# A block's MLP issued over four slots and a bit instead of ten

## The chip, the cores and the metric

The kernel runs on one core of a Trainium2 chip. The metric is the device time of one execution in microseconds. The engines of a core run their own instruction streams side by side and wait for each other on semaphores: TensorE (PE) does matmuls, VectorE (DVE), ScalarE (ACT) and GpSimd (POOL) work on tiles, and SyncE (SP) issues the transfers.

## What is computed

Attention with 4 batches, 8 heads, 576 positions and head size 64, in which each query keeps its 32 highest scores only, and behind it an MLP over 2304 tokens of width 512 with 2048 hidden values:

```python
scores = scale * np.matmul(q, k.transpose(0, 1, 3, 2))
kth = np.partition(scores, -top_k, axis=-1)[..., -top_k:-top_k + 1]
scores = np.where(scores >= kth, scores, -1000000000.0)
attn = np.exp(scores - max) ; attn = attn / (sum + 1e-09)
x = (attn @ v) of all heads side by side       # 2304 x 512
h = x @ w_in                                   # 2304 x 2048
g = h * np.tanh(log1p(exp(h)))                 # mish
y = g @ w_out                                  # 2304 x 512
```

## The kernel before

**Tiling.** The 2304 tokens are 18 blocks of 128 (`BLOCKS`). A block has four duos (`PPB`), each the 128 queries of two heads, so there are 72 duos (`DUOS`). The loops run over slots. In slot s each engine does one stage of several duos at once: PE computes `scores(s+2)` and transposes the finished weights of duo s-3 (`transposes`); ACT copies scores from PSUM (`copy_x(s+2)`), makes the penalty of duo s-1 (`penalties`), its exponentials (`exps`) and copies the transposed weights of duo s-3 (`copy_pT`); DVE does the whole `topk(s)` and one reciprocal (`inverse(s-2)`); POOL turns duo s-1's 32nd score into a limit (`negate`), subtracts (`exponents(s-1)`), adds 1e-9 to the sum (`guard`), multiplies the weights of duo s-2 by the reciprocal (`normalise`), and makes low parts of q and k (`split_q`, `split_k`). `values` of two duos (weights times v) stand together in every even slot. Blocks 4 and 13 are mixed: their 128 queries come from two batches, and their scores use all 128 rows of the array.

**The MLP of a block.** When its four duos are done, `copy_xT` brings x into SBUF; `up(m, j)`, j = 0 to 3, are 16 fp32 matmuls each (32 passes in a profile), written into two PSUM buffers in turn; `copy_up` moves a group to `g_raw`; `mish` works on each half; `split_g(m, h)` makes a rounded high part and a low part of a half (a cast and a subtraction on POOL); `down(m, j)` are 12 matmuls of 512 columns each; `copy_y` and `store` bring the result out. `ps_y` and `y_sb` are single.

**What sets the order.** Every engine's order is written out by hand, slot by slot, and each executes in that order. Before, `UP_SLOT` = 6 puts up(0, 0) in slot 6 and one further up into each slot; `MISH_SLOT` = 10 puts both halves of mish at the end of slot 10, 14, ...; the halves are split on POOL in the two slots after it; `DOWN_SLOT` = 12 puts one down group into each slot from 12 on. So a block's MLP stretches over slots 4m+6 to 4m+15. At slot 74 the slots end, and behind them stand down(15, 3), the last three ups, and the downs of blocks 16 and 17.

**Loads of new keys.** When a batch is done, `split_k` makes the high part of new keys on ACT and the low part on POOL at the end of slots 14, 15, 30 to 33, 50 and 51 (two in each of 14, 15, 50 and 51, one in the others).

Of the kernel before, what the change touches and what calls it, by code (L numbers as in the profile page):

```python
# [40 lines left out]

UP_SLOT, MISH_SLOT, DOWN_SLOT = 6, 10, 12
WCHUNKS = 8
# [59 lines left out]

STAGED = PPB


# [8 lines left out]
def program(nc, k_in, q_in, v, w_in, w_out, y_out):  # L115
    with ExitStack() as ctx:
# [77 lines left out]
        ghi_ready = sem("ghi_ready")  # L194
        glo_ready = sem("glo_ready")
        down_ready = sem("down_ready")
        y_copied = sem("y_copied")
# [23 lines left out]
        def _(sp):  # L221
# [51 lines left out]
            for k in range(KC):  # L273
                sp.dma_start(win[:, k, :], w_in[P * k:P * k + P, :]).then_inc(win_loaded, 16)
            for s in range(DUOS + DOWN_SLOT):
                if STAGED < s + 3 < DUOS:
                    load_q(s + 3)
                for c in w_chunks_at(s - 1):
                    if c + 2 < WCHUNKS:
                        load_w(c + 2)  # L280
                for g in splits_at(s - 1):
                    if PPB <= g and g + RAWS < PAIRS:
                        load_k(g + RAWS)
                for pr in range(PPB):
                    for i in range(1, len(V_USES[pr])):
                        if values_slot(V_USES[pr][i - 1][3]) == s:
                            load_v(pr, i)
                m, j = divmod(s - DOWN_SLOT, GROUPS)
                if j == GROUPS - 1 and 0 <= m < BLOCKS:
                    store(m)  # L290
# [3 lines left out]
        def _(pe):  # L294
# [82 lines left out]
            def down(m, j):  # L377
                if m == 0 and j == 0:
                    pe.wait_ge(wlo_ready, WCHUNKS)
                if j == 0 and m >= 1:  # L380
                    pe.wait_ge(y_copied, m)
                if j % 2 == 0:
                    pe.wait_ge(glo_ready, 2 * m + j // 2 + 1)
                for f in range(FPG * j, FPG * j + FPG):
                    for g, w in ((g_hi, w_hi), (g_hi, w_lo), (g_lo, w_hi)):
                        mm = pe.matmul(ps_y[:, :], g[:, f, :], w[:, f, :],  # L386
                                       start=(f == 0 and g is g_hi and w is w_hi), stop=(f == FT - 1 and g is g_lo),
                                       skip_group_check=True)
                mm.then_inc(down_ready, 1)

            pe.wait_ge(ident_ready, 1)
            for s in range(-2, DUOS + LAG_PT):
                if s >= LAG_PT:
                    transposes(s - LAG_PT)
                m, j = divmod(s - DOWN_SLOT, GROUPS)
                if m >= 0:
                    down(m, j)
                for d in (s - LAG_PT - 1, s - LAG_PT):
                    if d >= 0 and values_slot(d) == s:
                        values(d)  # L400
                if s + 2 < DUOS:
                    scores(s + 2)
                m, j = divmod(s - UP_SLOT, GROUPS)
                if m >= 0:
                    up(m, j)
            down(BLOCKS - 3, 3)
            for j in range(1, GROUPS):
                up(BLOCKS - 1, j)
            for j in range(GROUPS):
                down(BLOCKS - 2, j)  # L410
            for j in range(GROUPS):
                down(BLOCKS - 1, j)

        @block.scalar
        def _(act):
# [67 lines left out]
            def copy_up(m, j):  # L483
                n = GROUPS * m + j
                act.wait_ge(up_ready, n + 1)
                if n == 0:
                    act.wait_ge(wlo_ready, WCHUNKS)
                if j % 2 == 0 and m >= 1:

                    act.wait_ge(glo_ready, 2 * (m - 1) + j // 2 + 1)  # L490
                act.activation(g_raw[:, FPG * j:FPG * j + FPG, :], ps_u[:, n % 2, :, :],
                               ACT.Copy).then_inc(up_copied, 1)

            def mish(m):
                for h in range(2):
                    act.wait_ge(up_copied, GROUPS * m + 2 * h + 2)
                    g = g_raw[:, FT // 2 * h:FT // 2 * h + FT // 2, :]
                    act.activation(g, g, ACT.Mish).then_inc(mish_ready, 1)

# [8 lines left out]
            split_k(1)  # L508
            for s in range(-2, DUOS + LAG_PT):
                if s >= LAG_PT:  # L510
# [5 lines left out]
                m, j = divmod(s - UP_SLOT - 1, GROUPS)  # L516
                if m >= 0:
                    copy_up(m, j)
                if s >= LAG_PT and (s - LAG_PT) % PPB == PPB - 1:
                    copy_xT((s - LAG_PT) // PPB)  # L520
                if 0 <= s + 2 < DUOS:
                    copy_x(s + 2)
                m, j = divmod(s - DOWN_SLOT, GROUPS)
                if m >= 0 and j == GROUPS - 1:
                    copy_y(m)
                if 0 <= s - LAG_EXP < DUOS:
# [4 lines left out]
                for c in w_chunks_at(s):  # L531
                    split_w(c)
                m, j = divmod(s - MISH_SLOT, GROUPS)
                if m >= 0 and j == 0:
                    mish(m)
            copy_up(BLOCKS - 1, 0)
            copy_y(BLOCKS - 3)
            for j in range(1, GROUPS):
                copy_up(BLOCKS - 1, j)
            mish(BLOCKS - 1)  # L540
            copy_y(BLOCKS - 2)
            copy_y(BLOCKS - 1)

        @block.vector
        def _(dve):
# [4 lines left out]
            def topk(s):  # L550
# [8 lines left out]
                for r in range(TOPK // EIGHT - 1):  # L559
                    for t in range(2):  # L560
                        if r == 0:
                            dve.wait_ge(top8_ready, 2 * s + t + 1)
                        else:
# [4 lines left out]
                                          imm_value=NEG).then_inc(found, 1)  # L568
                    if r == 0 and s >= LAG_NORM:
                        inverse(s - LAG_NORM)  # L570
# [10 lines left out]
            for s in range(DUOS - LAG_NORM, DUOS):  # L581
                inverse(s)

        @block.gpsimd
        def _(pool):
# [57 lines left out]
            split_k(1)  # L643
            for s in range(-2, DUOS + LAG_NORM):
                if 0 <= s - LAG_EXP < DUOS:
                    negate(s - LAG_EXP)
                m, j = divmod(s - MISH_SLOT - 1, GROUPS)
                if m >= 0 and j < 2:
                    split_g(m, j)
                for c in w_chunks_at(s - 1):  # L650
                    split_w(c)
                if 0 <= s - LAG_NORM:
                    normalise(s - LAG_NORM)
                if 0 <= s - LAG_EXP < DUOS:
                    exponents(s - LAG_EXP)
                if s + 3 < DUOS:
                    split_q(s + 3)
                if 0 <= s - LAG_EXP < DUOS:
                    guard(s - LAG_EXP)
                if s > -2:  # L660
                    for g in splits_at(s):
                        split_k(g)
            for m in range(BLOCKS - 2, BLOCKS):
                for h in range(2):
                    split_g(m, h)

# [38 lines left out]
```

## Time and profile before

| | us |
|---|---|
| median of 3 runs | 783.95 (783.53 to 784.21) |
| profiled execution, device time | 782.78 |
| its span in the trace | 781.0 |
| PE busy | 717.6 (92%) |
| PE weight loads busy | 641.7 (82%) |
| DVE busy | 700.3 (90%) |
| ACT busy | 546.1 (70%) |
| POOL busy | 546.3 (70%) |

The span runs from the first to the last instruction of the trace, and the device time has some 1.8 us around it. The shares are averages over the whole span: DVE works only while there are duos, PE also behind them. So the slots (where both are busy) and the end (where only PE is) are to be read apart. The mean granted clock of PE over the profile is 0.986 of full speed.

### The profile page before, as it was taken

To read this page: it belongs to the slowest core of one execution; us is meant where nothing else is said; L and a number is where in the kernel's file an instruction comes from. 1 tells how busy PE (TensorE), PEld (TensorE's weight loads), DVE (VectorE), ACT (ScalarE), POOL (GpSimd) and SP (SyncE) were. 2 spreads that over 40 slices of the span, in tenths; PEclk is the share of its full clock that TensorE was granted. 3 is DMA by queue.
4 is the path that set the end of the run, shared out by engine and by line. 5 is a ranking of instruction groups with operands and counts; after the bars stand their busy time and mean duration, and the time that the engine had idled before them with its cause. 6 is when DMAs were issued, how large, how long until landed. Compare 5 with 4: busy or idle time off the path is not lost.

```text
span 781.0 us, 16741 instructions
## 1 busy us (share of the span) xinstructions
PE 717.6 (92%) x6280; PEld 641.7 (82%) x6280; DVE 700.3 (90%) x1513; ACT 546.1 (70%) x994; POOL 546.3 (70%) x677
## 2 busy tenths in 40 slices
PE   2257759999999999999999999999999999999998
PEld 2246758988888888888888888988888888889896
DVE  6999999998999999999999999998999999996000
ACT  4677666776868687878686878686868686867420
POOL 3977568697767676887676768687767776767333
PEclk9987999999999999999999999999999999999999
DMA  9521000031121000211100000020122000000000
GB/s 346 185 62 34 8 8 12 15 115 40 59 85 45 8 22 10 52 38 54 42 23 8 23 8 21 16 77 23 56 75 90 8 22 8 21 2 14 2 14 28
DMA packets 22689, 34.64 MB, mean 44 GB/s; under 512 B 2384, under 2 KB 11600, under 8 KB 22096
## 3 DMA queue, kind: packets, MB, share of 16 engines
q1 hardware_dynamic: 22608, 33.56, 13.4%
q8 instruction: 50, 0.82, 0.4%
q14 instruction: 31, 0.25, 0.1%
HBM read 28.84 MB, written 4.72 MB: 43 GB/s over the span
## 4 chain that ended last, share of the span: by engine, by line
PE 55%; DVE 32%; POOL 4%; ACT 4%; issue 4%; DMA 1%; SPq 0%; ACTq 0%; POOLq 0%
PE ps_u L373 22%; PE ps_y L386 16%; DVE left L565 15%; DVE top L573 12%; PE ps_s L314 5%; PE ps_s L332 5%; PE ps_o L357 5%; DVE top L558 5%; POOL p_sb L624 1%; PE ps_o L350 1%; ACT p_sb L464 1%; POOL g_lo L610 1%; ACT pT L473 1%; POOL p_sb L635 1%; POOL k_lo L588 1%
## 5 line engine op out<-in xcount | busy, mean ns | idle before, releaser
L573 DVE MAX8 top<-left 128x8 f32<-128x576 f32 x432 | 305.2, 751 | 0.0
L373 PE MATMUL ps_u<-xT,win 128*128 128x128 f32 x2304 | 275.6, 278 | 2.6 <-ACT xT L481 2.6
L373 PEld LDWEIGHTS ps_u<-xT,win 128*128 128x128 f32 x2304 | 263.9, 192 | 13.0 <-issue 9.2
L565 DVE MATCH_REPLACE8 left<-top,left 128x576 f32<-128x576 f32 x288 | 212.5, 748 | 0.0
L624 POOL TENSOR_TENSOR p_sb<-x_sb,p_sb 128x576 f32<-128x576 f32 x144 | 200.8, 1416 | 0.0
L464 ACT ACTIVATE p_sb<-p_sb,neg_max 128x576 f32<-128x576 f32 x144 | 111.3, 775 | 62.0 <-POOL p_sb L624 61.5
L635 POOL TENSOR_SCALAR p_sb<-p_sb,recip 128x576 f32<-128x576 f32 x144 | 106.2, 748 | 51.0 <-DVE recip L548 51.0
L386 PE MATMUL ps_y<-w_hi,g_hi 128*128 128x512 f32 x288 | 119.0, 413 | 0.7 <-ACT y_sb L504 0.7
L445 ACT ACTIVATE x_sb<-ps_s 128x576 f32<-128x576 f32 x144 | 85.6, 648 | 48.0 <-PE ps_s L314 47.8
L386 PE MATMUL ps_y<-w_hi,g_lo 128*128 128x512 f32 x288 | 113.0, 392 | 0.0
L386 PE MATMUL ps_y<-w_lo,g_hi 128*128 128x512 f32 x288 | 112.3, 390 | 0.0
L456 ACT ACTIVATE p_sb<-x_sb,limit 128x576 f32<-128x576 f32 x144 | 103.5, 770 | 8.2 <-POOL limit L615 8.2
L565 DVE MATCH_REPLACE8 left<-top,x_sb 128x576 f32<-128x576 f32 x144 | 106.3, 749 | 0.0
L558 DVE MAX8 top<-x_sb 128x8 f32<-128x576 f32 x144 | 101.4, 748 | 3.0 <-ACT x_sb L445 3.0
L473 ACT ACTIVATE pT<-ps_s 128x512 f32<-128x512 f32 (+1 forms) x144 | 84.6, 638 | 23.3 <-PE ps_s L332 23.3
L332 PE MATMUL ps_s<-ident,p_sb 128*128 128x128 f32 x648 | 85.7, 279 | 8.8 <-POOL p_sb L635 7.6
L610 POOL TENSOR_TENSOR g_lo<-g_raw,g_hi 128x1024 fp32r<-128x1024 f32 x36 | 86.0, 2389 | 3.1
L357 PEld LDWEIGHTS ps_o<-pT,v_sb 128*64 128x64 f32 x1280 | 72.0, 141 | 18.1 <-issue 13.7
L357 PE MATMUL ps_o<-pT,v_sb 128*64 128x128 f32 x1280 | 80.9, 282 | 6.1 <-ACT pT L473 6.1
L332 PEld LDWEIGHTS ps_s<-ident,p_sb 128*128 128x128 f32 x648 | 75.2, 144 | 10.4 <-ACT x_sb L445 5.9
L314 PE MATMUL ps_s<-k_hi,q_hi 64*128 64x288 f32 (+1 forms) x288 | 43.1, 362 | 42.1 <-ACT pT L473 21.4
L314 PEld LDWEIGHTS ps_s<-k_hi,q_hi 64*128 64x128 f32 (+1 forms) x288 | 25.5, 199 | 60.4 <-issue 43.6
(41 smaller groups left out, 730.1 us busy)
## 6 DMA issues: line engine op xcount, KB each, us to landing
v_sb<-v_in SPq DMA_DIRECT2D x32, 320.0 KB, 3.6
g_raw<-w_out SPq DMA_DIRECT2D x8, 512.0 KB, 3.8
win<-w_in SPq DMA_DIRECT2D x4, 1024.0 KB, 11.8
y_out<-y_sb SPq DMA_DIRECT2D x16, 256.0 KB, 2.0
k_raw<-k_in SPq DMA_DIRECT2D x14, 288.0 KB, 2.9
q_raw<-q_in SPq DMA_DIRECT2D x60, 64.0 KB, 1.8
q_raw<-q_in SPq DMA_DIRECT2D x8, 128.0 KB, 2.1
p_sb<-k_in SPq DMA_DIRECT2D x2, 288.0 KB, 5.2
```

The costliest lines, as they stand in the source:

```text
L314: mm = pe.matmul(ps_s[:, t, h, 0:HALF], q[r, s % QS, c:c + P], k[r, g % PPB, HALF * h:HALF * h + HALF], start=first, stop=final, skip_grou ...
L332: mm = pe.transpose(flat[:, P * k:P * k + P], p[:, P * k:P * k + P], ident[:, :])
L357: mm = pe.matmul(ps_o[D * h:D * h + D, j, :], v_sb[:, j, k, D * h:D * h + D], pT[:, s % 2, SPLIT_AT * h + k, :], start=(k == 0), stop=(k = ...
L373: mm = pe.matmul(ps_u[:, n % 2, i, :], win[:, k, P * f:P * f + P], xT[:, k, :], start=(k == 0), stop=(k == KC - 1), skip_group_check=True)
L386: mm = pe.matmul(ps_y[:, :], g[:, f, :], w[:, f, :], start=(f == 0 and g is g_hi and w is w_hi), stop=(f == FT - 1 and g is g_lo), skip_gr ...
L456: act.activation(p_sb[:, s % PS_, t, :], x_sb[:, s % XS, t, :], ACT.Relu, bias=limit[:, s % TS, t:t + 1], scale=-BLOW_UP).then_inc(penalty ...
L464: act.activation(p, p, ACT.Exp, bias=neg_max[:, s % TS, t:t + 1], scale=SCALE, accum_out=denom[:, s % TS, t:t + 1]).then_inc(exp_ready, 1)
L558: dve.max(best[:, t, 0:EIGHT], x[t]).then_inc(top8_ready, 1)
L565: dve.match_replace(out=left[:, t, :], in_to_replace=best[:, t, EIGHT * r:EIGHT * r + EIGHT], in_values=x[t] if r == 0 else left[:, t, :], ...
L573: dve.max(best[:, t, EIGHT * r + EIGHT:EIGHT * r + 2 * EIGHT], left[:, t, :]).then_inc(found, 1)
L624: pool.tensor_tensor(p, x_sb[:, s % XS, t, :], p, ALU.subtract).then_inc(arg_ready, 1)
L635: pool.tensor_scalar(p, p, recip[:, s % TS, t:t + 1], 1.0, ALU.mult, ALU.mult).then_inc(p_ready, 1)
```

## The change

The MLP of block m now takes slots 4m+6 to 4m+9 and the start of slot 4m+10. `mlp_at(s)` gives the block and its slot r, 0 to 3. PE does up 0 at the end of the first slot, up 1 and up 2 in the second, up 3 in the third, down 0, 1 and 2 in the fourth, and down 3 at the start of the next block's first slot. ACT copies groups 0 and 1 and does the first half's mish at the end of the second slot, copies groups 2 and 3 and does the other half's between `copy_x` and `exps` in the third. POOL splits one half in the third and one in the fourth slot. The second half of the last block is split on DVE, whose duos are done. On POOL, `guard` moves from the end of a slot to the start of the next one, and `normalise` stands behind `exponents` except in the third slot; on DVE `inverse` moves one pair of passes back. `copy_y`, `store` and the first waits on `w_out` are moved with them.

```diff
-UP_SLOT, MISH_SLOT, DOWN_SLOT = 6, 10, 12
+MLP_SLOT, MLP_SLOTS = 6, 4
+def mlp_at(s):
+
+    m, r = divmod(s - MLP_SLOT, MLP_SLOTS)
+    return (m if 0 <= m < BLOCKS else None), r
+SLOTS = MLP_SLOT + MLP_SLOTS * BLOCKS + 1
...
-            for s in range(-2, DUOS + LAG_PT):
-                if s >= LAG_PT:
+            for s in range(-2, SLOTS):
+                m, r = mlp_at(s)
+                before, last = mlp_at(s - 1)
+                if LAG_PT <= s < DUOS + LAG_PT:
                     transposes(s - LAG_PT)
-                m, j = divmod(s - DOWN_SLOT, GROUPS)
-                if m >= 0:
-                    down(m, j)
-                for d in (s - LAG_PT - 1, s - LAG_PT):
-                    if d >= 0 and values_slot(d) == s:
+                if before is not None and last == 3:
+                    down(before, 3)
+                if m is not None and r == 1:
+                    up(m, 1)
+                if m is not None and r == 2:
+                    up(m, 3)
+                if m is not None and r == 3:
+                    down(m, 0)
+                two = [d for d in (s - LAG_PT - 1, s - LAG_PT) if 0 <= d < DUOS and values_slot(d) == s]
+                if r != 2:
+                    for d in two:
                         values(d)
                 if s + 2 < DUOS:
                     scores(s + 2)
-                m, j = divmod(s - UP_SLOT, GROUPS)
-                if m >= 0:
-                    up(m, j)
-            down(BLOCKS - 3, 3)
-            for j in range(1, GROUPS):
-                up(BLOCKS - 1, j)
-            for j in range(GROUPS):
-                down(BLOCKS - 2, j)
-            for j in range(GROUPS):
-                down(BLOCKS - 1, j)
+                if r == 2:
+                    for d in two:
+                        values(d)
+                if m is not None and r == 0:
+                    up(m, 0)
+                if m is not None and r == 1:
+                    up(m, 2)
+                if m is not None and r == 3:
+                    down(m, 1)
+                    down(m, 2)
...
+                if before is not None and last == 3:
+                    copy_y(before)
+                if m is not None and r == 0:
+                    copy_xT(m)
+                if m is not None and r == 1:
+                    copy_up(m, 0)
+                    copy_up(m, 1)
+                    if s >= DUOS + LAG_PT:
+                        mish(m, 0)
+                if m is not None and r == 2:
+                    copy_up(m, 2)
+                    copy_up(m, 3)
                 if 0 <= s + 2 < DUOS:
                     copy_x(s + 2)
-                m, j = divmod(s - DOWN_SLOT, GROUPS)
-                if m >= 0 and j == GROUPS - 1:
-                    copy_y(m)
+                if m is not None and r == 2:
+                    mish(m, 1)
                 if 0 <= s - LAG_EXP < DUOS:
                     exps(s - LAG_EXP)
...
-                m, j = divmod(s - MISH_SLOT, GROUPS)
-                if m >= 0 and j == 0:
-                    mish(m)
...
+                if m is not None and r == 1 and s < DUOS + LAG_PT:
+                    mish(m, 0)
...
-                    if r == 0 and s >= LAG_NORM:
+                    if r == 1 and s >= LAG_NORM:
                         inverse(s - LAG_NORM)
...
+            g, f = BLOCKS - 1, slice(FT // 2, FT)
+            dve.wait_ge(mish_ready, 2 * g + 2)
+            dve.wait_ge(down_ready, GROUPS * g)
+            dve.tensor_copy(g_hi[:, f, :], g_raw[:, f, :]).then_inc(ghi_last, 1)
...
-                m, j = divmod(s - MISH_SLOT - 1, GROUPS)
-                if m >= 0 and j < 2:
-                    split_g(m, j)
+                if 0 <= s - LAG_NORM < DUOS:
+                    guard(s - LAG_NORM)
+                if m is not None and r == 2:
+                    split_g(m, 0)
+                if m is not None and r == 3 and m < BLOCKS - 1:
+                    split_g(m, 1)
                 for c in w_chunks_at(s - 1):
                     split_w(c)
-                if 0 <= s - LAG_NORM:
+                if r == 2 and 0 <= s - LAG_NORM < DUOS:
                     normalise(s - LAG_NORM)
                 if 0 <= s - LAG_EXP < DUOS:
                     exponents(s - LAG_EXP)
+                if r != 2 and 0 <= s - LAG_NORM < DUOS:
+                    normalise(s - LAG_NORM)
                 if s + 3 < DUOS:
                     split_q(s + 3)
-                if 0 <= s - LAG_EXP < DUOS:
-                    guard(s - LAG_EXP)
```

ACT, before: the slot in which both halves of mish stand, and the one behind it (`p_sb,denom` are the exponentials, `pT` the transposed weights, L491 copies an up group, L445 scores, L504 y).

```order
164 L491 ACTIVATE g_raw<-ps_u 128x512
165 L445 ACTIVATE x_sb<-ps_s 128x576 x2
166 L464 ACTIVATE p_sb,denom<-p_sb,neg_max 128x576 x2
...
182 L498 ACT_TABLE_LOAD
183 L498 ACTIVATE g_raw<-g_raw 128x1024 x2
184 L473 ACTIVATE pT<-ps_s 128x512
185 L473 ACTIVATE pT<-ps_s 128x640
186 L456 ACTIVATE p_sb<-x_sb,limit 128x576 x2
187 L434 ACTIVATE q_hi<-q_raw 128x128
188 L491 ACTIVATE g_raw<-ps_u 128x512
```

ACT, after: the end of a block's second slot and the whole third one (L523 is mish, L517 copies up groups, L470 scores, L489 the exponentials, L498 the transposed weights).

```order
190 L523 ACT_TABLE_LOAD
191 L523 ACTIVATE g_raw<-g_raw 128x1024
192 L498 ACTIVATE pT<-ps_s 128x512
193 L498 ACTIVATE pT<-ps_s 128x640
194 L481 ACTIVATE p_sb<-x_sb,limit 128x576 x2
195 L459 ACTIVATE q_hi<-q_raw 128x128
196 L517 ACTIVATE g_raw<-ps_u 128x512 x2
197 L470 ACTIVATE x_sb<-ps_s 128x576 x2
198 L523 ACTIVATE g_raw<-g_raw 128x1024
199 L489 ACT_TABLE_LOAD
200 L489 ACTIVATE p_sb,denom<-p_sb,neg_max 128x576 x2
```

One half of mish and the table load for the exponentials have moved between the copy of the scores and the exponentials of the third slot.

POOL, before: one of the two slots with a split of g (L608 and L610), then the start of the next (L635 is `normalise`, L624 `exponents`, L594 `split_q`, L628 `guard`, L615 and L617 `negate`).

```order
147 L615 TENSOR_SCALAR limit<-top 128x2
148 L617 TENSOR_SCALAR neg_max<-top 128x2
149 L608 CAST g_hi<-g_raw 128x1024
150 L610 TENSOR_TENSOR g_lo<-g_raw,g_hi 128x1024
151 L635 TENSOR_SCALAR p_sb<-p_sb,recip 128x576 x2
152 L624 TENSOR_TENSOR p_sb<-x_sb,p_sb 128x576 x2
153 L594 TENSOR_TENSOR q_lo<-q_raw,q_hi 128x128
154 L628 TENSOR_SCALAR denom<-denom 128x2
```

POOL, after: the fourth slot of a block (L648 and L650 are `negate`, L661 `guard`, L641 and L643 `split_g`, L657 `exponents`, L668 `normalise`, L627 `split_q`).

```order
156 L648 TENSOR_SCALAR limit<-top 128x2
157 L650 TENSOR_SCALAR neg_max<-top 128x2
158 L661 TENSOR_SCALAR denom<-denom 128x2
159 L641 CAST g_hi<-g_raw 128x1024
160 L643 TENSOR_TENSOR g_lo<-g_raw,g_hi 128x1024
161 L657 TENSOR_TENSOR p_sb<-x_sb,p_sb 128x576 x2
162 L668 TENSOR_SCALAR p_sb<-p_sb,recip 128x576 x2
163 L627 TENSOR_TENSOR q_lo<-q_raw,q_hi 128x128
```

`guard` (of the duo before) now stands ahead of the split, and `normalise` behind `exponents`.

DVE, after: its last instructions. Before, it ended with the two reciprocals.

```order
575 L598 MAX top<-left 128x8 x2
576 L573 RECIPROCAL recip<-denom 128x2 x2
577 L612 CAST g_hi<-g_raw 128x1024
578 L614 TENSOR_TENSOR g_lo<-g_raw,g_hi 128x1024
579 L127 UNCONDITIONAL_BRANCH
```

The split of the last half block has come behind them.

## Rows read from the trace of the kernel before

**Rows 1.** The page's chain that ended last; then DVE's longest wait (total, times, longest).

```profile
PE 55%; DVE 32%; POOL 4%; ACT 4%; issue 4%; DMA 1%; SPq 0%; ACTq 0%; POOLq 0%
...
DVE recip L548 <- POOL denom L628: 19.2, 7, 9.3
```

**Rows 2.** Timeline, PE, slots 67 and 68: start us, duration us, engine, line, operation, tiles.

```profile
667.98 1.15 PE L332 MATMUL ps_s<-ident,p_sb 128*128 128x128 f32 x9
...
671.83 0.53 PE L314 MATMUL ps_s<-k_hi,q_hi 64*128 64x288 f32 x4
...
672.82 3.84 PE L373 MATMUL ps_u<-xT,win 128*128 128x128 f32 x32
676.50 1.15 PE L332 MATMUL ps_s<-ident,p_sb 128*128 128x128 f32 x9
...
683.67 3.84 PE L373 MATMUL ps_u<-xT,win 128*128 128x128 f32 x32
687.34 1.15 PE L332 MATMUL ps_s<-ident,p_sb 128*128 128x128 f32 x9
```

**Rows 3.** Timeline, DVE: the first pass of topk in slots 9 and 10.

```profile
95.24 1.41 DVE L558 MAX8 top<-x_sb 128x8 f32<-128x576 f32 x2
104.94 1.41 DVE L558 MAX8 top<-x_sb 128x8 f32<-128x576 f32 x2
```

**Rows 4.** Timeline, PE, slots 11 and 12: idle time before an instruction in brackets.

```profile
117.62 0.70 PE L314 MATMUL ps_s<-k_hi,q_hi 64*128 64x288 f32 x4 [4.76 <-ACT pT L473]
...
123.83 1.15 PE L332 MATMUL ps_s<-ident,p_sb 128*128 128x128 f32 x9
```

**Rows 5.** The end: PE enters slot 70; the last copy of y.

```profile
695.86 1.15 PE L332 MATMUL ps_s<-ident,p_sb 128*128 128x128 f32 x9
...
777.97 0.60 ACT L504 ACTIVATE y_sb<-ps_y 128x512 f32<-128x512 f32 x1 [11.26 <-PE ps_y L386]
```

**Rows 6.** The chain in order of time: one down group.

```profile
124.98 2.76 PE ps_y L386 x12
```

**Rows 7.** Timeline, PE, slot 51: scores of a mixed block, and the up behind them.

```profile
513.94 0.77 PE L314 MATMUL ps_s<-k_hi,q_hi 128*128 128x288 f32 x4 [0.96 <-ACT pT L473]
...
515.65 3.73 PE L373 MATMUL ps_u<-xT,win 128*128 128x128 f32 x32
```

**Rows 8.** Timeline, slot 30: scores, their copies on ACT, the exponentials.

```profile
308.87 0.53 PE L314 MATMUL ps_s<-k_hi,q_hi 64*128 64x288 f32 x4
...
309.96 1.19 ACT L445 ACTIVATE x_sb<-ps_s 128x576 f32<-128x576 f32 x2 [0.38 <-PE ps_s L314]
...
311.04 0.78 ACT L464 ACTIVATE p_sb<-p_sb,neg_max 128x576 f32<-128x576 f32 x1
```

**Rows 9.** Timeline, ACT, slots 10 and 11: both halves of mish, the table load, exponentials.

```profile
114.40 2.00 ACT L498 ACTIVATE g_raw<-g_raw 128x1024 f32<-128x1024 f32 x2
...
121.92 1.28 ACT L464 ACT_TABLE_LOAD   x1 [1.12 <-POOL p_sb L624]
123.21 0.78 ACT L464 ACTIVATE p_sb<-p_sb,neg_max 128x576 f32<-128x576 f32 x1
```

**Rows 10.** Timeline, POOL, slot 11: split of g, normalise, exponents, split of q, guard.

```profile
115.52 1.04 POOL L608 CAST g_hi<-g_raw 128x1024 fp32r<-128x1024 f32 x1 [0.18 <-ACT g_raw L498]
...
119.00 1.47 POOL L635 TENSOR_SCALAR p_sb<-p_sb,recip 128x576 f32<-128x576 f32 x2
120.44 2.77 POOL L624 TENSOR_TENSOR p_sb<-x_sb,p_sb 128x576 f32<-128x576 f32 x2
123.17 0.46 POOL L594 TENSOR_TENSOR q_lo<-q_raw,q_hi 128x128 fp32r<-128x128 f32 x1
124.93 0.22 POOL L628 TENSOR_SCALAR denom<-denom 128x2 f32<-128x2 f32 x1 [1.30 <-ACT p_sb L464]
```

**Rows 11.** Timeline, slot 30: the split of new keys on ACT and POOL.

```profile
312.55 0.68 ACT L424 ACTIVATE k_hi<-k_raw 128x576 fp32r<-128x576 f32 x1
...
313.31 1.41 POOL L588 TENSOR_TENSOR k_lo<-k_raw,k_hi 128x576 fp32r<-128x576 f32 x1 [0.34 <-ACT k_hi L424]
```

More of the change, by code:

```diff
@@ L195, in program @@
         glo_ready = sem("glo_ready")
+        ghi_last = sem("ghi_last")
+        glo_last = sem("glo_last")
         down_ready = sem("down_ready")
@@ L274, in _ @@
                 sp.dma_start(win[:, k, :], w_in[P * k:P * k + P, :]).then_inc(win_loaded, 16)
-            for s in range(DUOS + DOWN_SLOT):
+            for s in range(SLOTS + 1):
                 if STAGED < s + 3 < DUOS:
@@ L287, in _ @@
                             load_v(pr, i)
-                m, j = divmod(s - DOWN_SLOT, GROUPS)
-                if j == GROUPS - 1 and 0 <= m < BLOCKS:
+                m, r = mlp_at(s - 1)
+                if m is not None and r == 3:
                     store(m)
@@ L381, in down @@
                     pe.wait_ge(y_copied, m)
-                if j % 2 == 0:
+                if j == 2 and m == BLOCKS - 1:
+                    pe.wait_ge(glo_last, 1)
+                elif j % 2 == 0:
                     pe.wait_ge(glo_ready, 2 * m + j // 2 + 1)
@@ L402, in _ @@
                     scores(s + 2)
-                m, j = divmod(s - UP_SLOT, GROUPS)
-                if m >= 0:
-                    up(m, j)
-            down(BLOCKS - 3, 3)
-            for j in range(1, GROUPS):
-                up(BLOCKS - 1, j)
-            for j in range(GROUPS):
-                down(BLOCKS - 2, j)
-            for j in range(GROUPS):
-                down(BLOCKS - 1, j)
+                if r == 2:
[5 more added lines that the diff above has]
+                    up(m, 2)
+                if m is not None and r == 3:
+                    down(m, 1)
+                    down(m, 2)
         @block.scalar
@@ L485, in copy_up @@
                 act.wait_ge(up_ready, n + 1)
-                if n == 0:
-                    act.wait_ge(wlo_ready, WCHUNKS)
+                if m == 0 and j % 2 == 0:
+                    act.wait_ge(wlo_ready, WCHUNKS - 1 + j // 2)
                 if j % 2 == 0 and m >= 1:
@@ L492, in copy_up, with mish @@
                                ACT.Copy).then_inc(up_copied, 1)
[L494 to L498, printed above, removed]
+            def mish(m, h):
+                act.wait_ge(up_copied, GROUPS * m + 2 * h + 2)
+                g = g_raw[:, FT // 2 * h:FT // 2 * h + FT // 2, :]
+                act.activation(g, g, ACT.Mish).then_inc(mish_ready, 1)
             def copy_y(m):
@@ L508, in _ @@
             split_k(1)
-            for s in range(-2, DUOS + LAG_PT):
-                if s >= LAG_PT:
+            for s in range(-2, SLOTS):
+                m, r = mlp_at(s)
+                before, last = mlp_at(s - 1)
+                if LAG_PT <= s < DUOS + LAG_PT:
                     copy_pT(s - LAG_PT)
@@ L515, in _ @@
                     split_q(s + 3)
[L516 to L520, printed above, removed]
+                if before is not None and last == 3:
[10 more added lines that the diff above has]
+                    copy_up(m, 3)
                 if 0 <= s + 2 < DUOS:
                     copy_x(s + 2)
-                m, j = divmod(s - DOWN_SLOT, GROUPS)
-                if m >= 0 and j == GROUPS - 1:
-                    copy_y(m)
+                if m is not None and r == 2:
+                    mish(m, 1)
                 if 0 <= s - LAG_EXP < DUOS:
@@ L532, in _ @@
                     split_w(c)
-                m, j = divmod(s - MISH_SLOT, GROUPS)
-                if m >= 0 and j == 0:
-                    mish(m)
[L536 to L542, printed above, removed]
+                if m is not None and r == 1 and s < DUOS + LAG_PT:
+                    mish(m, 0)
         @block.vector
@@ L582, in _ @@
                 inverse(s)
+            g, f = BLOCKS - 1, slice(FT // 2, FT)
+            dve.wait_ge(mish_ready, 2 * g + 2)
+            dve.wait_ge(down_ready, GROUPS * g)
+            dve.tensor_copy(g_hi[:, f, :], g_raw[:, f, :]).then_inc(ghi_last, 1)
+            dve.wait_ge(ghi_last, 1)
+            dve.tensor_tensor(g_lo[:, f, :], g_raw[:, f, :], g_hi[:, f, :].bitcast(F32),
+                              ALU.subtract).then_inc(glo_last, 1)
         @block.gpsimd
@@ L643, in _ @@
             split_k(1)
-            for s in range(-2, DUOS + LAG_NORM):
+            for s in range(-2, SLOTS):
+                m, r = mlp_at(s)
                 if 0 <= s - LAG_EXP < DUOS:
                     negate(s - LAG_EXP)
-                m, j = divmod(s - MISH_SLOT - 1, GROUPS)
-                if m >= 0 and j < 2:
-                    split_g(m, j)
+                if 0 <= s - LAG_NORM < DUOS:
[4 more added lines that the diff above has]
+                    split_g(m, 1)
                 for c in w_chunks_at(s - 1):
                     split_w(c)
-                if 0 <= s - LAG_NORM:
+                if r == 2 and 0 <= s - LAG_NORM < DUOS:
                     normalise(s - LAG_NORM)
@@ L662, in _ @@
                         split_k(g)
-            for m in range(BLOCKS - 2, BLOCKS):
-                for h in range(2):
-                    split_g(m, h)
 def kernel(q, k, v, moe_w_in, moe_w_out):
```

## The prediction

> **What bounds the kernel now.** I read the chain that ended last first [rows 1]: 55% PE and 32% DVE. Two engines share the bound, so the next thing to look at is their step. DVE starts a new duo every 9.70 us (104.94 - 95.24) [rows 3] and needs no pause between passes. PE, in a slot pair near the end, takes 687.34 - 667.98 = 19.36 us for two slots [rows 2], or 9.68 a slot. Both are full. DVE's wait for the reciprocal's input is 19.2 us in 7 waits, the longest (9.3) behind its last duo, so about 10 us lie among the duos [rows 1]. Then the end: PE enters slot 70 at 695.86, and y is copied for the last time at 777.97 [rows 5], which is 82.1 us of PE work with no topk beside most of it. The start is different: PE does no down group before slot 12, entered at 123.83, and waited 4.76 us in slot 11 [rows 4].
>
> So PE is the resource. The change takes no PE work away. It can gain only by filling PE's idle time before slot 12 and by avoiding later waits. It loses wherever its new order makes PE wait.
>
> **PE's pieces** from the same rows. A down group is 2.76 [rows 6]. Transposes are 671.83 - 667.98 - 2.76 = 1.09, scores 672.82 - 671.83 = 0.99, an up group 676.50 - 672.82 = 3.68, and values with scores 683.67 - 676.50 - 1.09 - 2.76 = 3.32, so values are 2.33 [rows 2].
>
> The slots of a block are then, in the new order: first 1.09 + 2.76 + 3.32 + 3.68 = 10.85; second 1.09 + 3.68 + 0.99 + 3.68 = 9.44; third 1.09 + 3.68 + 0.99 + 2.33 = 8.09; fourth 1.09 + 0.99 + 3 x 2.76 = 10.36. Sum 38.74, against 38.72 now and 38.80 of DVE. Per block nothing is gained or lost by itself. Check on before: slots 12 to 69 are 29 pairs, 561.4; eight scores of mixed blocks take 515.65 - 513.94 = 1.71 instead of 0.99 [rows 7], 5.8 more; PE's span there is 695.86 - 123.83 = 572.0, so some 4.8 us in 58 slots are waits. That is small: before, PE hardly waits in the slots.
>
> **The start.** In the new order PE enters slot 10 when POOL has normalised duo 7 in slot 9. From the start of slot 8 on DVE (95.24 - 9.70 = 85.54): the reciprocal stands behind 4 of 7 pairs of passes, 9.70 x 4/7 = 5.54, with itself 5.75; normalise 1.44; exponents 2.73, that is 9.9; the second exponential, with the way to guard, some 1.0; then guard 0.3, split of g 119.00 - 115.52 = 3.48, exponents 2.73, normalise 1.47 and 0.1 to the release [rows 10]. Sum 19.0, so slot 10 starts at 104.6; I take 104.8. With 3 down groups done by then, PE has work from there on.
>
> **The waits that the order brings.** This is the term that I am least sure of, so it is worked out step by step, from PE's entry into a block's third slot (0) to its entry into the next first slot. PE itself needs 8.09 + 10.36 = 18.45. The other way is through ACT and POOL:
> - up 3 and transposes, 4.77; scores start; the copy on ACT starts 309.96 - 308.87 = 1.09 later, 5.86; 311.04 - 309.96 = 1.08 for both copies, 6.94 [rows 8];
> - the half of mish that now stands there, 2.00 / 2 = 1.00, then the table load 123.21 - 121.92 = 1.29, 9.23 [rows 9];
> - from the first exponential to guard 124.93 - 123.21 = 1.72, 10.95 [rows 9, 10];
> - guard 0.3, which now stands ahead of the split and so holds POOL's whole fourth slot; split 3.48; exponents 2.73; normalise 1.47; release 0.1: 19.03 [rows 10].
>
> PE's transposes wait for that normalise. So PE loses 19.03 - 18.45 = 0.58 us per block. The same sum for the fourth slot's scores, which need the copied transposes (10.7 + 1.2 against 8.09 + 3.85), comes out even, and down 2, needing the second split at 14.7 against 15.7, doesn't wait. The 15 blocks from slot 10 to slot 70 pay it, less the two in which the longer mixed scores cover it: 13 x 0.58 = 7.5. Its bounds: below, nothing, since a sum of eleven durations can be off by 0.5 and some work may overlap more than in the rows; above, 1.2 per block if each hand-over costs a little more.
>
> **New keys.** Before, splits of keys fell on slots with a split of g. Now slots 14, 15, 30, 31, 50 and 51 have none. Only slot 32, a third one, is hit: POOL finishes its split of q at 9.6, waits for ACT's copy of the keys, which comes behind the exponentials (10.8 + 0.6), then works 1.41 [rows 11], to 12.9; negate and guard 0.9, and 3.48 + 2.73 + 1.57 give 21.6, against 18.45: 3.15, of which 0.58 is counted, so 2.6. The bounds are 0 and 4.
>
> **The end.** From slot 70 on PE has 8 up groups before and after, and 9 down groups (1, 3, 1, 4) instead of 14 (5 in slots 70 to 74, and 9): 5 x 2.76 = 13.8 less. The wait for the copy of y between the last two blocks, 0.7, goes as well. 82.1 - 14.5 = 67.6. New waits there: down 0 of the last block needs mish and split of the first half (copy 0.6, load 1.3, mish 1.0, split 3.5, together 6.4 behind up 1), while up 2 and up 3 cover 7.4; the other half needs 0.6 + 1.0 and two passes on DVE, some 2.4 by its 9.70 / 14 = 0.69 per 576 columns, covered by down 0 and 1 (5.5). Nothing is late there; without cover it would be 1 to 2 us. Slots 72 to 74 have no scores or exponents beside them, and POOL's sum is shorter than PE's. The stores keep their place behind copy_y.
>
> **Other edits at nothing.** The reciprocal, 2.8 us later, delays normalise; DVE itself is helped, since guard may come 2.8 us later before it waits. In a first or second slot normalise then ends some 7.4 us after DVE's start, more than 2 us before PE wants it. The number of table loads goes from 34 to 36, the same two a block; the last slots' are under PE's work. Transfers don't come earlier or later by more than a slot, and none is in the chain but 1%.
>
> **A rule against the change.** The rows show a switch of tables as 1.28 us, and the exponential begins 1.29 after the load began [rows 9]. The Trainium skill, ScalarE: Activation LUTs, section "What ACT_TABLE_LOAD costs", gives a load of about 1283 ns and a drain of about 1380 ns besides. The trace agrees on the first and shows no second part. It matters since the load now lies in the path that I summed.
>
> **Sum.** 104.8 + 15 x 38.72 (580.8) + mixed 5.8 + 7.5 + 2.6 = 701.5 at slot 70; + 67.6 = 769.1 at the last copy of y, against 777.97. The span ended 781.0 - 777.97 = 3.0 later: 772.1. The device time of the profiled execution is 1.8 above its span: 773.9. The median of the runs is 1.2 above that execution (783.95 - 782.78): **775.1**.
>
> **Rivals.**
> - *PE runs through* (27%). The chain above is shorter than PE's own 18.45, and nothing of 7.5 and 2.6 is paid: 765.0, and up to 770.5 with half of it. For it: the difference is only 0.58 in 19. Against it: before, behind slot 50 with mish and key splits together, PE already waited 0.96 us for ACT's copy of the transposes [rows 7].
> - *The chain as summed* (53%): 770.5 to 779.
> - *The chain is longer* (13% for 779 to 785.5, of which 4% lie within 0.2% of before; 7% beyond). The same guard-to-normalise chain in the third and fourth slot, with a price per block P instead of 0.58: the time is 765.0 + 2.6 + 13 P, and it passes 783.95 at P = 1.26, that is 0.7 us more in the chain than summed. It could come from ACT: in a second slot its copies, exponentials, load and mish end 4.77 + 1.09 + 1.08 + 1.72 + 1.29 + 1.00 = 10.95 after PE's entry, 1.5 behind PE's entry into the third [rows 8, 9, 10]. My estimate is that it catches up with some 0.7 us to spare; if it does not, all that I started from PE's scores starts later. An engine drain at each load, as long as the load itself, would be such a thing: 1.3 us in the chain, 14 times, and 775.1 + 18.2 = 793.3. No row shows one [rows 9], so I give it 1% of the 7. The Trainium skill, in the section named above, states such a drain.
>
> Slower beyond 0.2% is then 7%, same 4% and faster 89%. A measurement of this kernel can tell about 0.2%, 1.6 us, from no change. The range that holds 8 in 10: from 766 to 781; below it some 5%, above it 14%.
>
> **What would show it.** Right: PE enters the transposes of slot 10 near 105 and shows 12 down passes ahead of it; PE's transposes in each first slot show an idle time of about 0.6 released by POOL's normalise; DVE's last pass still ends near 716, since PE, and not DVE, sets the step; the time from slot 70 to the last copy of y is 67 to 69. The whole gain is then in the end, 14.5, less some 6 that slot 70 comes later than before. Wrong: PE has no idle time in the slots and slot 70 starts before 694 (first rival); or the waits at a block's first slot are over 1.2 and slot 70 starts after 708; or PE waits in the last block, between up 3 and down 0, which would mean that its cover is not there.

## The result and the profile after

| | before | after |
|---|---|---|
| median of 5 runs, us | 783.75 (783.03 to 784.21) | 779.51 (779.38 to 779.93) |
| profiled execution, device time | 782.78 | 779.93 |
| its span | 781.0 | 777.9 |
| PE enters slot 10 | 99.88 | 105.58 |
| PE enters slot 70 | 695.86 | 706.35 |
| last copy of y begins | 777.97 | 774.93 |

The ratio is 0.9948, with a 95% interval from 0.9933 to 0.9962. The change makes the kernel 4.2 us faster. The forecast was 8.9 us, so the sign and the range held, and the size was off by more than a factor of two.

The chain that ended last, on the page of the changed kernel, answers to [rows 1]:

```profile
PE 40%; POOL 34%; DVE 10%; ACT 10%; issue 5%; DMA 0%; ACTq 0%; SPq 0%; POOLq 0%
PE ps_u L386 16%; POOL p_sb L657 11%; POOL g_lo L643 10%; PE ps_y L401 9%; POOL p_sb L668 6%; DVE left L590 5%; PE ps_s L327 5%; PE ps_o L370 5%; PE ps_s L345 4%; POOL g_hi L641 4%; DVE top L598 4%; ACT p_sb L489 3%; ACT L523 2%; ACT g_raw L523 2%; DVE top L583 2%
```

POOL had 4% of the chain before and has 34% now. Its lines are the subtraction (L657), the split of g (L641, L643) and the normalising (L668): the work of a block's fourth slot. The waits of PE between slot 10 and slot 70 (for whom: total, times, longest) show the same:

```profile
PE ps_s L327 <- ACT pT L498: 6.7, 13, 1.5
PE ps_s L345 <- POOL p_sb L668: 5.6, 13, 1.3
PE ps_y L401 <- POOL g_lo L643: 0.8, 1, 0.8
```

PE waits 13.1 us there, against 4.8 between slots 12 and 70 before. One ordinary block, slots 46 to 50, in PE's timeline (start us, duration us, engine, line, operation, tiles, idle time before it):

```profile
466.65 1.18 PE L345 MATMUL ps_s<-ident,p_sb 128*128 128x128 f32 x9 [0.34 <-POOL p_sb L668]
477.49 1.15 PE L345 MATMUL ps_s<-ident,p_sb 128*128 128x128 f32 x9
486.81 1.15 PE L345 MATMUL ps_s<-ident,p_sb 128*128 128x128 f32 x9
494.78 1.20 PE L345 MATMUL ps_s<-ident,p_sb 128*128 128x128 f32 x9
498.94 0.53 PE L327 MATMUL ps_s<-k_hi,q_hi 64*128 64x288 f32 x4 [0.22 <-ACT pT L498]
506.03 1.17 PE L345 MATMUL ps_s<-ident,p_sb 128*128 128x128 f32 x9 [0.36 <-POOL p_sb L668]
```

The block takes 506.03 - 466.65 = 39.38 us. It would be 38.72 by [rows 2]. The first, second and third slot take 10.84, 9.32 and 7.97, none longer than in the sum; the fourth takes 11.25, and both idle times stand in or behind it. What ACT and POOL do in these microseconds:

```profile
493.63 1.06 ACT L523 ACTIVATE g_raw<-g_raw 128x1024 f32<-128x1024 f32 x1
494.80 1.28 ACT L489 ACT_TABLE_LOAD   x1
496.10 0.78 ACT L489 ACTIVATE p_sb<-p_sb,neg_max 128x576 f32<-128x576 f32 x1
...
497.63 1.17 ACT L498 ACTIVATE pT<-ps_s 128x512 f32<-128x512 f32 x2
```

```profile
497.81 0.22 POOL L661 TENSOR_SCALAR denom<-denom 128x2 f32<-128x2 f32 x1 [0.67 <-ACT p_sb L489]
498.09 1.04 POOL L641 CAST g_hi<-g_raw 128x1024 fp32r<-128x1024 f32 x1
499.21 2.42 POOL L643 TENSOR_TENSOR g_lo<-g_raw,g_hi 128x1024 fp32r<-128x1024 f32 x1
501.57 2.84 POOL L657 TENSOR_TENSOR p_sb<-x_sb,p_sb 128x576 f32<-128x576 f32 x2
504.38 1.50 POOL L668 TENSOR_SCALAR p_sb<-p_sb,recip 128x576 f32<-128x576 f32 x2
```

Mish, load, exponentials, guard (L661, after an idle time of 0.67), split, subtraction, normalise: 504.38 + 1.50 = 505.88, and PE's transposes begin at 506.03. It is the chain of the prediction, piece for piece: 506.03 - 486.81 = 19.22 us from PE's third slot on, 19.03 in the sum.

Two theories of the lost gain went to the chip. **A**: this chain over ACT and POOL, with normalise at its end, holds PE once a block. **B**: PE's and DVE's own steps set the pace, and the idle times would turn up elsewhere if they were removed; for the moved guard and reciprocal, B says that they are what makes four slots possible.

### The profile page after: what moved, and what is told of

Same layout as the page of the kernel before. It is cut to its first block, busy times and chain, and to the rows that moved or that the text cites. A ratio compares the mean times of both kernels' runs of the same rounds, so it can differ in the third digit from the quotient of the medians.

```text
span 777.9 us, 16744 instructions
## 1 busy us (share of the span) xinstructions
PE 715.6 (92%) x6280; PEld 642.4 (83%) x6280; DVE 703.2 (90%) x1515; ACT 552.8 (71%) x996; POOL 546.7 (70%) x675
## 3 DMA queue, kind: packets, MB, share of 16 engines
q1 hardware_dynamic: 22608, 33.56, 13.5%
## 4 chain that ended last, share of the span: by engine, by line
PE 40%; POOL 34%; DVE 10%; ACT 10%; issue 5%; DMA 0%; ACTq 0%; SPq 0%; POOLq 0%
PE ps_u L386 16%; POOL p_sb L657 11%; POOL g_lo L643 10%; PE ps_y L401 9%; POOL p_sb L668 6%; DVE left L590 5%; PE ps_s L327 5%; PE ps_o L370 5%; PE ps_s L345 4%; POOL g_hi L641 4%; DVE top L598 4%; ACT p_sb L489 3%; ACT L523 2%; ACT g_raw L523 2%; DVE top L583 2%
## 5 line engine op out<-in xcount | busy, mean ns | idle before, releaser
L386 PE MATMUL ps_u<-xT,win 128*128 128x128 f32 x2304 | 271.4, 276 | 1.4 <-ACT xT L506 1.4
L657 POOL TENSOR_TENSOR p_sb<-x_sb,p_sb 128x576 f32<-128x576 f32 x144 | 202.3, 1428 | 66.6 <-ACT p_sb L481 66.6
L489 ACT ACTIVATE p_sb<-p_sb,neg_max 128x576 f32<-128x576 f32 x144 | 110.8, 774 | 46.9 <-POOL p_sb L657 46.7
L498 ACT ACTIVATE pT<-ps_s 128x512 f32<-128x512 f32 (+1 forms) x144 | 85.4, 642 | 57.1 <-PE ps_s L345 57.1
L401 PE MATMUL ps_y<-w_hi,g_hi 128*128 128x512 f32 x288 | 117.2, 407 | 1.6 <-POOL g_lo L643 1.6
L668 POOL TENSOR_SCALAR p_sb<-p_sb,recip 128x576 f32<-128x576 f32 x144 | 106.9, 756 | 3.6 <-DVE recip L573 3.6
L470 ACT ACTIVATE x_sb<-ps_s 128x576 f32<-128x576 f32 x144 | 85.6, 647 | 26.4 <-PE ps_s L327 26.3
L643 POOL TENSOR_TENSOR g_lo<-g_raw,g_hi 128x1024 fp32r<-128x1024 f32 x35 | 83.8, 2393 | 3.0
L327 PE MATMUL ps_s<-k_hi,q_hi 64*128 64x288 f32 (+1 forms) x288 | 43.0, 359 | 34.6 <-ACT pT L498 14.5
L641 POOL CAST g_hi<-g_raw 128x1024 fp32r<-128x1024 f32 x35 | 36.4, 1039 | 47.2 <-ACT g_raw L523 45.8
```

Source lines behind the costliest of these rows:

```text
L386: mm = pe.matmul(ps_u[:, n % 2, i, :], win[:, k, P * f:P * f + P], xT[:, k, :], start=(k == 0), stop=(k == KC - 1), skip_group_check=True)
L401: mm = pe.matmul(ps_y[:, :], g[:, f, :], w[:, f, :], start=(f == 0 and g is g_hi and w is w_hi), stop=(f == FT - 1 and g is g_lo), skip_gr ...
L489: act.activation(p, p, ACT.Exp, bias=neg_max[:, s % TS, t:t + 1], scale=SCALE, accum_out=denom[:, s % TS, t:t + 1]).then_inc(exp_ready, 1)
L643: pool.tensor_tensor(g_lo[:, f, :], g_raw[:, f, :], g_hi[:, f, :].bitcast(F32), ALU.subtract).then_inc(glo_ready, 1)
L657: pool.tensor_tensor(p, x_sb[:, s % XS, t, :], p, ALU.subtract).then_inc(arg_ready, 1)
L668: pool.tensor_scalar(p, p, recip[:, s % TS, t:t + 1], 1.0, ALU.mult, ALU.mult).then_inc(p_ready, 1)
```

## Experiments

All are edits of the changed kernel. Each time is a median; block is PE's time from the first slot of an ordinary block to the next.

| run | us | block, us |
|---|---|---|
| changed kernel | 779.51 | 39.38 |
| x1_norm_first | 771.41 | 38.85 |
| x2_keys_later | 777.07 | 39.38 |
| x3_old_guard | 768.77 | 38.86 |
| x4_no_tables | 767.47 | 38.55 |
| x5_cast_twice | 798.67 | 40.48 |
| x8_guard_only | 783.63 | 39.85 |
| x7_guard_keys | 768.02 | 38.86 |
| x9_early_load | 766.03 | 38.83 |

**Normalise ahead of the subtraction in the fourth slot.**

```diff
-                if r == 2 and 0 <= s - LAG_NORM < DUOS:
+                if r >= 2 and 0 <= s - LAG_NORM < DUOS:
                     normalise(s - LAG_NORM)
...
-                if r != 2 and 0 <= s - LAG_NORM < DUOS:
+                if r < 2 and 0 <= s - LAG_NORM < DUOS:
                     normalise(s - LAG_NORM)
```

> Of the changed kernel, one edit: in a block's fourth slot POOL normalises before it subtracts (as in the third). Theory A, the chain over ACT and POOL holds PE back once per block: the normalise that PE's next transposes wait for ends 2.8 us earlier, the wait of 0.36 us at each block's first slot goes (and the 1.30 at slot 34), the 0.22 at the fourth slot's scores stays; a block goes from 39.38 to about 38.9 us, slot 70 starts some 7 us earlier, near 699, and the time is about 773. Theory B, the slot times are set by PE and DVE themselves and these idle times only show slack that exists anyway: the wait turns up somewhere else, blocks stay at 39.4 and the time within 1 us of 779.5.

Measured: 771.41 us (771.22 to 771.87), ratio to before 0.984 (0.9827 to 0.9854). PE's waits between slot 10 and the end are now:

```profile
PE ps_s L327 <- ACT pT L498: 6.5, 13, 1.5
PE ps_y L401 <- POOL g_lo L643: 1.6, 2, 0.8
PE ps_u L386 <- ACT xT L506: 1.4, 2, 0.7
```

The waits for POOL's normalise (L668) are gone, and none has taken their place; those for ACT have stayed, as A said. Slot 70 starts at 697.67 instead of 706.35. B falls: 8.1 us hang on two lines of POOL's order. A block takes 38.85 us, as A said, and the time is 1.6 below its 773.

**The opposite: more of the same.** The cast of the fourth slot's split done twice.

```diff
+                if h == 1:
+                    pool.tensor_copy(g_hi[:, f, :], g_raw[:, f, :]).then_inc(cast_done, 1)
+                    pool.wait_ge(cast_done, m + 1)
                 pool.tensor_copy(g_hi[:, f, :], g_raw[:, f, :]).then_inc(ghi_ready, 1)
```

> Of the changed kernel, with the cast of the split in a block's fourth slot done twice on POOL, 1.12 us more behind the guard. Theory A, that slot's POOL work stands in the chain with no slack: each block gets about 1.1 us longer (39.38 to 40.5), the two mixed ones 0.8, about 17 us in all, 796.5. Theory B, PE's wait shows slack on POOL: less than half of it arrives, under 788.

Measured: 798.67 us (797.82 to 799.38), 19.2 more than the changed kernel. PE's first slots of blocks 9 and 10:

```profile
436.71 1.17 PE L346 MATMUL ps_s<-ident,p_sb 128*128 128x128 f32 x9 [1.32 <-POOL p_sb L672]
...
477.19 1.18 PE L346 MATMUL ps_s<-ident,p_sb 128*128 128x128 f32 x9 [1.32 <-POOL p_sb L672]
```

A block takes 40.48, and 1.10 of the 1.12 us arrive. So there is no slack in POOL's fourth slot. B falls. The total is 2 us above what A said. Down 2 in slot 73 waits 1.0 us longer than in the changed kernel (1.85 against 0.83), and the rest is not traced to a place.

**Keys.** The split of the new keys that fell on a third slot.

```diff
 SPLIT_SLOT = {g: g - 3 if g < PPB else LAST_USE[g - PPB] - 2 for g in range(PAIRS)}
+SPLIT_SLOT[10] = 33
```

> Of the changed kernel, one edit: the split of pair 10's keys moves from slot 32 (a block's third) to slot 33. Theory A: the waits of block 6 (1.41 at the scores, 0.81 at down 2, 1.30 at the next transposes) shrink to those of the other blocks, the block from 42.64 to about 39.4 us, and the time is about 776.3. Theory B: POOL and ACT do the same work in four slots, so the block keeps at least half of it; 778.5 to 779.5.

Measured: 777.07 us (776.79 to 777.56), 2.4 less. Block 6 goes from 348.49 - 305.85 = 42.64 to 345.67 - 305.70 = 39.97, so most of its excess is gone, as A said, with 0.6 left. The time is 0.8 above A's 776.3.

**The old order of guard, normalise and reciprocal, under the new placing of the MLP.**

```diff
@@ VectorE
-                    if r == 1 and s >= LAG_NORM:
+                    if r == 0 and s >= LAG_NORM:
                         inverse(s - LAG_NORM)
@@ GpSimd
-                if 0 <= s - LAG_NORM < DUOS:
-                    guard(s - LAG_NORM)
...
-                if r == 2 and 0 <= s - LAG_NORM < DUOS:
+                if 0 <= s - LAG_NORM < DUOS:
                     normalise(s - LAG_NORM)
                 if 0 <= s - LAG_EXP < DUOS:
                     exponents(s - LAG_EXP)
-                if r != 2 and 0 <= s - LAG_NORM < DUOS:
-                    normalise(s - LAG_NORM)
                 if s + 3 < DUOS:
                     split_q(s + 3)
+                if 0 <= s - LAG_EXP < DUOS:
+                    guard(s - LAG_EXP)
```

> Of the changed kernel, undone: guard stands again at the end of POOL's slot, normalise ahead of exponents in every slot, and the reciprocal after DVE's first replace pair. What is left is the new placing of the MLP alone. Theory A: PE's transposes wait for a normalise that now ends earlier, so the waits at the first slot go; but DVE's reciprocal comes 2.8 us earlier in its slot and must wait for a guard behind exponentials that the half of mish and the table load delay, about 3 us after PE enters the fourth slot, so DVE waits once a block and stays closely behind PE. PE is the bound with about 38.9 us a block and the time 773 to 777. Theory B, the moved guard and reciprocal are what lets four slots work: without them DVE's waits hold everything, over 40 us a block and over 788.

Measured: 768.77 us (768.67 to 768.83), ratio to before 0.9806 (0.9792 to 0.9819). That is below the range of both theories, and 10.7 us faster than the changed kernel. The placing of the MLP alone is worth 15 us, and the reordering that came with it gives back most. A had PE's block right (38.86 us against its 38.9), but expected DVE to wait once a block. The guard at the end of POOL's slot 48, and DVE's slot 49, in which the reciprocal needs it:

```profile
489.78 0.22 POOL L661 TENSOR_SCALAR denom<-denom 128x2 f32<-128x2 f32 x1 [1.30 <-ACT p_sb L489]
```

```profile
487.33 1.41 DVE L583 MAX8 top<-x_sb 128x8 f32<-128x576 f32 x2
490.10 0.17 DVE L573 RECIPROCAL recip<-denom 128x2 f32<-128x2 f32 x1
```

PE entered slot 49 at 486.76, and guard starts 3.0 us later, as computed. But DVE had entered its slot only at 487.33 and reaches the reciprocal at 490.10, 0.1 us after guard ends at 490.00. The old order is on time by a hair in ordinary blocks. The margin that the moved guard and reciprocal were to bring shows in no run: DVE's waits for guard are 16.8 us in 7 waits here and 19.5 in 8 in x1_norm_first (10.5 and 11.0 of them behind the last duo), and a mixed block takes 42.1 us here against 42.6 there.

**Only guard and reciprocal undone.** As the last one, but normalise stays behind the subtraction except in the third slot.

> Of the changed kernel, undone: guard stands again at the end of POOL's slot, and the reciprocal after DVE's first replace pair; normalise stays behind exponents except in the third slot. Theory A, it is the place of normalise behind the split and the exponents that holds PE: guard at the slot's end makes that chain 0.5 us longer (from guard to the cast 0.77 us instead of 0.28), blocks 39.9, the time about 786. Theory C, the moved guard and reciprocal are what cost: blocks at 38.9 and under 773, like the kernel in which all three were undone.

Measured: 783.63 us (783.43 to 784.13). Blocks are 39.85 (468.17 - 428.32), as A said; the total is 2.4 less than its 786. Theory C falls. The late normalise is the costly part, and it costs more under the old guard (783.63 - 768.77 = 14.9 us against 8.1, though x8_guard_only and x3_old_guard differ in a block's first and second slot as well): beside it the moved guard and reciprocal are worth 4 us. With normalise first again they are not needed: x3_old_guard, in which all of it is undone, is 2.6 us faster than x1_norm_first.

**No table loads.**

```diff
-                act.activation(g, g, ACT.Mish).then_inc(mish_ready, 1)
+                act.activation(g, g, ACT.Relu).then_inc(mish_ready, 1)
```

> Of the changed kernel, with relu in the place of mish (so the MLP's nonlinearity is left out), which takes as long and needs no other table: it takes out the table loads alone, 36 of them down to 1. Theory A: the load of 1.28 us stands in the chain from PE's third slot to the next first slot, so both waits (0.22 and 0.36) go in every block, and the 1.54 us of slots 9, 17 and 53 fall to about 0.3: blocks at about 38.8, the time 769 to 771. Theory B: as many waits turn up elsewhere and the time stays above 777.

Measured: 767.47 us (767.27 to 767.73). Half a block of relu takes 1.06 us on ACT as half a block of mish did, and one table load is left of 36. No ordinary block shows a wait on PE, and a block takes 38.55 (497.98 - 459.43). The gain is a little more than A's. One number of A was wrong: the 1.54 us of slots 9, 17 and 53 fell to 0.84, not to 0.3. So table loads make only half of that wait.

**Keys later, under the old order.** Both edits above together.

> The new placing of the MLP with the old order of guard, normalise and reciprocal (768.8), and the split of pair 10's keys moved from slot 32 to slot 33. Theory A: block 6 goes from 40.7 to about 38.9 us: 767.0. Theory B: PE and DVE are both at their bound in this kernel (38.85 and 38.80 us a block), so nothing is gained: 768.8.

Measured: 768.02 us (768.01 to 768.19), 0.75 less, between the two. Block 6 goes from 40.68 to 39.42 (340.74 - 301.32), but the next block shows a new wait of 1.01 us for ACT's copy of x:

```profile
348.97 3.84 PE L387 MATMUL ps_u<-xT,win 128*128 128x128 f32 x32 [1.01 <-ACT xT L507]
```

**The table load before the wait.** In four blocks a one-column exponential behind mish, so that ACT loads the table at once.

```diff
                 if m is not None and r == 2:
                     mish(m, 1)
+                    if m == 0:
+                        act.wait_ge(ident_ready, 1)
+                    if m in (0, 2, 11, 16):
+                        act.activation(spare[:, m:m + 1], ident[:, 0:1], ACT.Exp)
```

> The kernel with both edits (expected at 767.0), and in four blocks (0, 2, 11, 16) an exponential of one column behind the third slot's half of mish. It makes ACT load the table at once, where the load stood behind the wait for POOL. If that load is what makes the wait of 1.2 to 1.5 us in slots 9, 17 and 53, these go, and the 0.8 in slot 73 nearly: about 3.5 us less than without, 763.5. If DVE's pace is the bound by then, less than 1.5 us.

Measured: 766.03 us (765.93 to 766.23), ratio to before 0.9777 (0.9762 to 0.9791), and 2.0 less than without it. ACT in slot 16 of the changed kernel, and of this one:

```profile
173.53 1.09 ACT L523 ACTIVATE g_raw<-g_raw 128x1024 f32<-128x1024 f32 x1
176.28 1.28 ACT L489 ACT_TABLE_LOAD   x1 [1.65 <-POOL p_sb L657]
177.57 0.78 ACT L489 ACTIVATE p_sb<-p_sb,neg_max 128x576 f32<-128x576 f32 x1
```

```profile
170.82 1.09 ACT L525 ACTIVATE g_raw<-g_raw 128x1024 f32<-128x1024 f32 x1
171.93 1.28 ACT L564 ACT_TABLE_LOAD   x1
173.23 0.20 ACT L564 ACTIVATE spare<-ident 128x1 f32<-128x1 f32 x1
173.34 0.76 ACT L491 ACTIVATE p_sb<-p_sb,neg_max 128x576 f32<-128x576 f32 x1
```

In the changed kernel the load stood behind the wait for POOL (in x7_guard_keys it did too, for 1.20 us); now it runs in that time. PE's waits in slots 9, 17 and 53 fall from 1.53, 1.19 and 1.21 to 0.84, 0.50 and 0.50, by 0.7 each, and the 0.84 in slot 73 goes. The rest of the three waits stays, so the gain is 2.0 and not 3.5 us; PE starts slot 10 0.88 us earlier, but in slot 13, where nothing was put in, its wait grows from 0.21 to 0.88. This is the fastest kernel of the study: 17.4 us below the kernel before (783.45 us in these runs), 13.5 below the changed one.

## Why the prediction was off

The mechanism, the sign and the range were right. The forecast gain was twice too large, because five terms of the sum were each too small, all in the same direction. **The step that failed most** is the waits of the two blocks with mixed scores (PE's slots 14 to 17 and 50 to 53). The sum put them at nothing, on the ground that the longer scores cover them; the trace has a wait of 1.54 us in each, and this term is off by 2.0 us. Behind it, and behind the misses of the start, the keys and the end, stands in part one assumption of the chain: "the half of mish, then the table load", with the exponential's input ready. In five slots (8, 16, 32, 52 and 72) it was not ready, and the load stood still until POOL had delivered. [rows 9] had such a wait, of 1.12 us, ahead of the load; I read only the load's length from it. The five terms:

- **Start.** Slot 10 at 105.58 instead of 104.8: 0.8. In slot 8 the exponentials' load waited 1.48 us for POOL's first subtraction, where I had let it overlap. x9_early_load, in which it doesn't wait, enters slot 10 0.88 us earlier than x7_guard_keys.
- **Ordinary blocks.** 12 of them take 39.41 on average instead of 39.30: 1.3. Two larger misses nearly cancel here, which is luck. Without waits the block is 38.55 (x4_no_tables), not 38.72; and the waits cost 39.38 - 38.55 = 0.83, not 0.58. The idle times of 0.22 and 0.36 that the profile shows add up to my 0.58, but they are read too short. The profile gives the last down matmul 0.39 us, while its successor can begin 0.24 us after its start. PE's entry into slot 50, in the changed kernel and without table loads:

```profile
505.28 0.39 PE L401 MATMUL ps_y<-w_hi,g_lo 128*128 128x512 f32 x1
506.03 1.17 PE L345 MATMUL ps_s<-ident,p_sb 128*128 128x128 f32 x9 [0.36 <-POOL p_sb L668]
```

```profile
497.74 0.39 PE L401 MATMUL ps_y<-w_hi,g_lo 128*128 128x512 f32 x1
497.98 1.14 PE L345 MATMUL ps_s<-ident,p_sb 128*128 128x128 f32 x9
```

From start to start that is 0.75 against 0.24, a loss of 0.51 us for 0.36 of idle time. At the fourth slot's scores it is 0.61 against 0.32, a loss of 0.29 for 0.22. The sum of both is 0.80 of the 0.83.

- **Mixed blocks.** 42.62 and 42.59 instead of 41.6: 2.0, the largest miss. The longer scores do cover the wait at the next block's first slot. But the fourth slot's scores wait 1.54 us. POOL and PE in slots 15 to 17:

```profile
166.04 2.80 POOL L621 TENSOR_TENSOR k_lo<-k_raw,k_hi 128x576 fp32r<-128x576 f32 x2 [0.79 <-ACT k_hi L449]
174.76 2.83 POOL L657 TENSOR_TENSOR p_sb<-x_sb,p_sb 128x576 f32<-128x576 f32 x2
180.42 0.77 PE L327 MATMUL ps_s<-k_hi,q_hi 128*128 128x288 f32 x4 [1.54 <-ACT pT L498]
```

Two keys are split in the slot before the third. POOL's subtraction begins 174.76 - 166.22 = 8.54 us after PE's entry into the third slot, against 493.30 - 486.81 = 6.49 in slot 48, and the table load starts only when its first half is there. Of the 1.54 us, 0.84 stay without any table load (x4_no_tables) and 0.7 are the load's. That the splits of the keys make POOL late is read from its order in the trace; no run moved these four splits. The miss is less than the wait, since PE's own pieces were some 0.5 us a block shorter than in the sum.

- **Keys.** Block 6 took 42.64 instead of 41.9: 0.7; in slot 32 the load waited for POOL as well, by 0.73 us. Its excess over an ordinary block is 42.64 - 39.38 = 3.26, where I had 2.6, and x2_keys_later removes 2.67 of it.
- **The end.** 774.93 - 706.35 = 68.6 instead of 67.6: the "nothing is late there" failed in slot 73, where down 2 waited 0.83 us for its split, behind a table load that had waited 1.11 us for POOL. The last block's own cover (up 2 and up 3 over the first half, down 0 and 1 over the second) held.

These are 5.8 us of span (777.9 against 772.1). What the place of the load alone is worth, in the start, the mixed blocks and the end together, is measured in x9_early_load (under the old order): 2.0 us. The device time of the median lies 1.6 above the span of the profile here, not 3.0, which takes 1.4 off: 4.4 us, 779.5 against 775.1.

**What held.** The chain was named with its length (19.0, measured 19.2), and x5_cast_twice shows that what is added to it reaches PE nearly whole (1.10 of 1.12 us a block). Shortening it by 2.8 us, in x1_norm_first, gave 0.53 a block: then it is shorter than PE's own work. The gain of the end, 14.5, measured 82.1 - 68.6 = 13.5. DVE's last pass ended near 722 instead of 716, dragged along by PE.

**The rivals.** "PE runs through", with 765.0 to 770.5 us, is what x3_old_guard comes to (768.8), and nearly x1_norm_first (771.4). In the changed kernel the chain is longer than PE's work in every ordinary block; with normalise first 8.1 us of its distance go, and the mixed blocks, the keys and the end make the rest. A drain beside each table load is shown by no row: in slot 48 mish ends at 493.63 + 1.06 = 494.69, the load begins at 494.80 and the exponential at 496.10, 1.30 us after the load began. The Trainium skill, ScalarE: Activation LUTs, section "What ACT_TABLE_LOAD costs", has such a drain beside each load; the measurement decides, and the forecast was right to leave it out.

**The point that I missed altogether** is not a term of the sum but a question. I costed the changed order of guard and normalise as given, wrote that normalise behind the subtraction ends in time in the first two slots, and never summed the fourth slot with the old order. By the same durations it is 2.7 us shorter with normalise first, some 2 us less than PE needs, and that was 8 of the 15 us that the new placing is worth.

## What to carry to other kernels

When two engines are both full (here 38.6 and 38.8 us a block), a helper engine's order can decide: put first what the full engine waits for, even if the work behind it comes later. A change that moves several things can hold a gain and a loss side by side: here the placing gave 15 us and the reordering took 10.7 back, and only undoing one of them showed it. An activation of another table behind a wait on another engine carried its table load behind that wait too (1.65 us idle, then 1.28 of load); a one-column activation ahead of the wait brought the load into the idle time.

## What the runs showed of the hardware that I had not expected

A table load waits with its activation: in slot 16 ACT stood idle for 1.65 us and the load then took 1.28, instead of running in that time. The kernel before had shown it already, with 1.12 us ahead of the load in [rows 9]. And idle times of PE of 0.22 and 0.36 us in the profile cost 0.83 us a block, when the kernels with and without them are compared.
